# Four reorderings in a fused attention, expert and mixer kernel: GpSimd's splits, the stores of u, one sum of weights, the first means

## The reference, cut to what matters

```python
# 1. attention, 8 heads, 768 tokens, 64 per head: a window of 16 plus 24 block summaries
k_sum = k.reshape(B, H, nb, block, D).max(axis=3)
v_sum = v.reshape(B, H, nb, block, D).mean(axis=3)
a = softmax([masked scale*q@k.T, scale*q@k_sum.T + log(block)])
x = a @ [v, v_sum]
# 2. mixture of 4 experts, each a causal attention of width 64; top 2 by a gate
logits = x @ w_gate;  w = softmax over the two largest
out += w[e] * (softmax(causal(scale * q_e @ k_e.T)) @ v_e @ wo[e])
# 3. mixer
u   = x + (relu(x.T @ w_tok1) @ w_tok2).T
out = u + relu(u @ w_ch1) @ w_ch2
```

## Time and profile before

| what | value |
|---|---|
| median of 3 runs | 450.01 us |
| the profiled execution | 449.9 us, of which the profile spans 448.1 us |
| PE busy | 430.1 us (96%) |
| DVE, ACT, POOL busy | 298.0, 227.8, 134.9 us |
| chain that ended last | PE 85%, DVE 8%, ACT 3%, issue 3% |
| granted clock of PE | 1.00 in every stretch |
| PE idle, 0 to 157 us | 12.75 us |
| PE idle, 157 to 262 us | 1.95 us |

### The profile page before, as it was taken

The page is one execution under the profiler, slowest core; times in us unless marked ns, Lnnn a source line. Parts: engine busy times, 40 slices in busy tenths (PEclk is TensorE's granted clock), DMA queues, the critical chain, the costliest instruction groups (busy, mean ns, idle before and its releaser), DMA issues.

```text
span 448.1 us, 8624 instructions
## 1 busy us (share of the span) xinstructions
PE 430.1 (96%) x3332; PEld 365.2 (81%) x3332; DVE 298.0 (67%) x549; ACT 227.8 (51%) x591; POOL 134.9 (30%) x170
## 2 busy tenths in 40 slices
PE   8889998998997999999999999999999999999997
PEld 3668996787775699968876898988998898989885
DVE  4983489776477834797766977676775775475353
ACT  5884647765247945777783462444442243233120
POOL 3797683000016412000268155632132022200000
PEclk9999999999999999999999999999999999999999
DMA  8964074000582230000033111132123063201103
GB/s 280 345 205 137 3 217 171 1 2 0 187 332 66 50 119 1 0 1 1 1 96 101 41 48 47 48 94 73 41 77 94 1 234 94 78 18 48 47 1 142
DMA packets 14370, 39.69 MB, mean 89 GB/s; under 512 B 1608, under 2 KB 2552, under 8 KB 14328
## 3 DMA queue, kind: packets, MB, share of 16 engines
q1 hardware_dynamic: 13464, 37.55, 25.5%
q10 hardware_dynamic: 864, 1.57, 0.9%
HBM read 33.56 MB, written 4.72 MB: 85 GB/s over the span
## 4 chain that ended last, share of the span: by engine, by line
PE 85%; DVE 8%; ACT 3%; issue 3%; POOL 0%; ACTq 0%; DVEq 0%; POOLq 0%
PE ps_s L690 35%; PE ps_o L690 19%; PE ps_x L690 14%; PE ps_t L690 10%; PE ps_t L862 4%; PE ps_t L757 2%; ACT PA L1101 1%; DVE nmaxM L1451 1%; DVE nmaxA L1359 1%; PE ps_x L876 1%; DVE QS L1399 0%; DVE PTA L1379 0%; DVE PTM L1462 0%; DVE gate_gt L1431 0%; PE ps_s L943 0%
## 5 line engine op out<-in xcount | busy, mean ns | idle before, releaser
L1339 ACT ACTIVATE HID_h<-HID_raw 128x384 fp32r<-128x384 f32 x48 | 25.1, 526 | 72.2 <-DVE HID_raw L1667 32.0
L639 POOL TENSOR_TENSOR W_raw<-W_raw 128x256 f32<-128x256 f32 x11 | 11.7, 1059 | 98.9 <-DMA W_raw<-in_ch 88.2
L1101 ACT ACTIVATE PA<-ps_s,biasA 128x120 f32<-128x120 f32 x96 | 33.6, 377 | 12.7 <-DVE biasA L1363 9.8
L553 POOL TENSOR_TENSOR PA<-PA,denA 128x480 f32<-128x480 f32 x24 | 23.7, 987 | 46.7 <-DVE denA L1372 46.7
L690 PE MATMUL ps_s<-C_h,HID_l 128*128 128x512 f32 x96 | 37.7, 393 | 0.0
L690 PE MATMUL ps_s<-C_l,HID_h 128*128 128x512 f32 x96 | 37.7, 393 | 0.0
L690 PE MATMUL ps_s<-C_h,HID_h 128*128 128x512 f32 x96 | 37.6, 392 | 0.0
L1165 ACT ACTIVATE PM<-ps_s,nmaxM 128x128 f32<-128x128 f32 (+5 forms) x48 | 30.1, 634 | 9.7 <-DVE nmaxM L1451 9.3
L1656 DVE SCALAR_TENSOR_TENSOR HID_l<-HID_raw,HID_h 128x384 fp32r<-128x384 f32 x48 | 28.0, 586 | 10.4 <-ACT HID_h L1339 8.1
L690 PE MATMUL ps_o<-V_h,W_h 128*128 128x384 f32 x96 | 32.8, 342 | 0.1
L690 PE MATMUL ps_o<-V_h,W_l 128*128 128x384 f32 x96 | 32.4, 337 | 0.0
(11 more groups left out here) (255 smaller groups left out, 1265.4 us busy)
## 6 DMA issues: line engine op xcount, KB each, us to landing
VW<-in_vw SPq DMA_DIRECT2D x12, 512.0 KB, 8.3
W_raw<-in_ch SPq DMA_DIRECT2D x12, 512.0 KB, 3.5
C_raw<-in_ch SPq DMA_DIRECT2D x12, 512.0 KB, 3.9
KP<-in_kT SPq DMA_DIRECT2D x8, 384.0 KB, 6.9
VT<-in_vT SPq DMA_DIRECT2D x8, 384.0 KB, 7.3
out_x<-US SPq DMA_DIRECT2D x12, 256.0 KB, 2.1
QT<-in_qT SPq DMA_DIRECT2D x7, 384.0 KB, 6.8
raw<-in_tok SPq DMA_DIRECT2D x4, 384.0 KB, 3.2
```

The lines of the kernel that those rows point to most:

```text
L553: pool.tensor_tensor(PA[:, u % NPA, :, :], PA[:, u % NPA, :, :], denA[:, u % 2, 1, :].unsqueeze(2).broadcast_to([P, 4, KC]), ALU.mult).the ...
L639: pool.tensor_tensor(W[S3], W[A11], W[A21], ALU.subtract).then_inc(w_sum, 1)
L1101: last = act.activation(PA[:, u % NPA, j, :], ps_s[u % 2][:, j % 2, (j // 2) * KC:(j // 2 + 1) * KC], ACT.Exp, bias=biasA[:, u % 4, j:j + ...
L1339: act.activation(*own(s, n, half), ACT.Relu).then_inc(g_hi, 1)
```

## The change

Four edits, none of which adds or removes arithmetic:

1. GpSimd makes splits 3 and 4 (wo, first half of w_tok1) ahead of `no_lows`; splits 5 and 6 stay behind it, and the last split, 7, waits in addition for the whole gate (`m_g` at 12).
2. The six stores of u are issued by SP, among its other DMAs; ACT no longer issues them. Batch 1's `place_means(b, 0, 1)` and `(b, 0, 2)` stand ahead of the fifth store, the three of the second half behind the last.
3. Of the four sums of weights on VectorE the fourth moves behind the low part of the last x.
4. The first means of batch 0 move behind the transposes of unit 0 on PE, and behind the copy of its transposes on ACT.

```diff
+N_EARLY = 5
@@ SP
+            def store_u(b, t):
+                sp.wait_ge(m_u, b * TQ + (t + 1))
+                sp.dma_start(u_d[t * P:(t + 1) * P, :], US1[t][:, :]).then_inc(st_u[t], 16)
...
-                for q in range(2):
-                    for i in range(1 - q, 3):
-                        place_means(b, q, i)
+                for t in range(TQ):
+                    if t == TQ - 2:
+                        for i in (1, 2):
+                            place_means(b, 0, i)
+                    store_u(b - 1, t)
+                for i in range(3):
+                    place_means(b, 1, i)
@@ GpSimd
                 if b == 0:
-                    pool.wait_ge(c_lo, 3)
+                    pool.wait_ge(c_lo, N_EARLY)
...
                 if b == 0:
-                    split(len(PACED))
+                    for n in range(len(PACED), N_EARLY):
+                        split(n)
                 no_lows(b)
                 if b == 0:
-                    for n in range(len(PACED) + 1, N_TOK2):
+                    for n in range(N_EARLY, N_TOK2):
+                        if n == N_TOK2 - 1:
+                            pool.wait_ge(m_g, NGATE)
                         split(n)
@@ PE
+                    if k <= NU + 2:
+                        a_transpose(b, k - 3)
                     if b == 0 and k == 3:
                         a_first_means(b)
-                    if k <= NU + 2:
-                        a_transpose(b, k - 3)
@@ ACT
-            def store_u(b, t):
-                act.wait_ge(m_u, b * TQ + (t + 1))
-                act.dma_start(u_d[t * P:(t + 1) * P, :], US1[t][:, :]).then_inc(st_u[t], 16)
...
+                    if 3 <= k <= NU + 2:
+                        a_to_sbuf(b, k - 3)
                     if b == 0 and k == 3:
                         a_first_means(b)
-                    if 3 <= k <= NU + 2:
-                        a_to_sbuf(b, k - 3)
...
                 for t in range(TQ):
-                    if more:
-                        store_u(b, t)
@@ DVE
                 dve.tensor_tensor(W[S2], W[S1], W[A11], ALU.subtract).then_inc(w_sum1, 1)
+
+            def last_row_sum():
+                W = [W_raw[1][:, a, :, :] for a in range(NB7)]
                 dve.wait_ge(w_sum1, 3)
                 dve.tensor_tensor(W[S4], W[A12], W[S2], ALU.subtract).then_inc(w_sum1, 1)
...
                 if not more:
                     second_row_sums()
                 m_x2_lo(b, TQ - 1)
+                if not more:
+                    last_row_sum()
```

## The result

| what | before | after |
|---|---|---|
| median | 450.01 us | 446.11 us (4 runs, 445.61 to 446.54) |
| ratio, with its 95% interval | | 0.9901 (0.9883 to 0.9919) |
| profiled execution, its span | 449.9, 448.1 us | 445.93, 444.1 us |

By the medians the changed kernel is faster by 3.9 us; the forecast was 3.1. Its median is 0.1 us inside the low end of the range (446.0 to 448.3), while the ratio, applied to 450.01, gives 445.55, a saving of 4.5 us (3.6 to 5.3), just outside that end. The next lines are from the page of the changed kernel: part 1 (busy us, share, count) and, from part 3, the DMA queue of SP. The arithmetic is as before; ACT's queue has no line any more.

A forecast was written before the change was run, and what follows sets the result against it. PE, busy 96% of the span, was taken to bound the kernel. Savings of 1.30 + 1.10 + 0.75 + 0 = 3.15 us off 450.0 gave 446.9 us, with a range of 446.0 to 448.3 us.

The forecast's parts named there:

- Part 1: GpSimd's splits around the gate of batch 0: gate's last instruction 3.90 us earlier, 1.30 us reach PE; bounds 0.6 and 1.7.
- the margin of 1.0 us: Ahead of batch 0's gate: GpSimd's split 6 ends at 57.1 us, the gate starts at 58.08, clear by 1.0.
- The bound of 1.7: Upper bound of the 1.30 us at batch 0's gate, if batch 1's four extra transposes were inside its 14.00 us.
- the four additional transposes of batch 1: Transposes of u on PE, only in batch 1's 14.00 us stretch, compared with batch 0's 15.30 us.
- Part 2: Stores of u off ACT's queue: at the change of batch `normalise` of unit 2 comes 1.10 us earlier; bounds 0.3 and 1.28.
- The rival in which the next wait catches it: Change of batch: full VectorE and GpSimd queues hold unit 3 back, 0.3 of 1.10 arrives, 447.7 us; chance 0.10.
- the stores landing late: Slower rival: u's stores land like SP's loads, `normalise` of unit 2 comes 4.54 us late, 452.5 us; chance 0.02.
- Part 3: VectorE's fourth sum, last x of batch 1: low part starts earlier, PE gains 0.75 us; bounds 0.4 and 0.79.
- Part 4: First means of batch 0: transposes fill PE's 0.67 us gap, VectorE's queue is full; gain 0, bounds -0.3 and 0.3.
- The port lock, a cost of 0: Splits 3 and 4 at 42 to 48.5 us beside VectorE instructions reading PSUM lose nothing to locked ports.
- The stores behind SP's loads, a cost of 0: Stores of u in SP's queue behind batch 1's loads of values: landings as before, 2.0 to 6.1 us after issue.

## Why the prediction was right, and where it was wrong

- **Bound and method.** Right. PE bounds the kernel, each saving was carried to the end once made, and the running difference has no step from 74 to 126 us.
- **Part 1, 1.30 us.** Right in mechanism and size for that execution (1.30, 1.29 and 1.36 in three traces). Two details were off: the margin of 1.0 us was 0.04 where the start came early, and the wait for the gate does nothing. The bound of 1.7 was too low: I took the four additional transposes of batch 1 as the only uncertainty of the 1.30, while the stall itself moves with the phase of two engines, 1.25 to 2.0 us of PE in four traces of the old order.
- **Part 2, 1.10 us.** Right: 1.06. The rival in which the next wait catches it didn't come, nor the stores landing late.
- **Part 3, 0.75 us** measured 0.75 and 0.73. **Part 4, 0** measured 0, for the reason given: VectorE's queue.
- **The port lock, a cost of 0** for the splits moved beside other work of VectorE: right, the running difference doesn't move there. **The stores behind SP's loads, a cost of 0**: right, but from rows read too widely, as said at part 2.
- **The step that failed** is the first one, before any part. PE's gaps were listed "besides the start", which put the start at nothing without a reason, and then came "that is 0.1 us under the median of the runs, so a saving worked out in this trace is taken off 450.0", and with it the range. An execution near the median isn't typical in each of its stretches: this one started late (8.22 us; mean of 14: 7.77), held by fillers that took 6.75 us, and had a cheap stall at the gate (1.30; mean of four: 1.49). The savings themselves were 3.15 us in its own terms and the trace after shows 3.19 for them. What the profiled execution has above that is the start, 0.75 us, for which the sum had no term and the range no room.
- **How far this explains the medians** is argued, not shown, since only a profiled execution shows its start. Three medians of the changed kernel stood 3.9, 3.07 and 3.74 us under those of the kernel before beside them: with the same parts, the size that is measured moves by 0.8 us. The base moved as well: 450.01 came from 3 runs, and later medians of the same kernel were 449.75, 449.65 and 449.91, 0.24 us lower in the mean. An estimate with that base, the counted 3.15 and 0.19 for the dearer stalls gives 446.4, against 446.29 for the mean of the changed kernel's three medians; the 446.11 of the first is luck of its few executions, as far as these runs tell. The likeliest time could not have been known better than by some 0.4 us, and a range whose low end stood 0.9 us under the forecast, all used up by known mechanisms, was too narrow by about that much.

What stays open: what sets the landing of the second load of keys and the moment at which the fillers speed up, and whether the mean saving of the three comparisons, 3.6 us, is above the counted 3.15 by more than chance. Dearer stalls of the old order at the gate would give some 0.2 of it. The first scores start at 7.64 us in the mean of the eight profiles with most of the change and at 7.95 in the other six, a difference that so few profiles with a spread of 1.1 us don't settle.

## What to carry to other kernels

Where two builds run the same matmuls in the same order, subtract the starts of like matmuls: each step of the difference is a place to look for one cause, and what lies in front of the first edited instruction is not the edit's. There, ask what the first useful instruction waits for in each trace: here it was PE's own fillers in one profile and a load in the next. Take the range of a small change from the spread of executions too, at the start and wherever two engines contend by phase, and not from the mechanisms alone. And look behind a gap before closing it: moving GpSimd's maxima gained nothing until VectorE, next in line, had room.

## What the runs showed of the hardware

- The second load of keys lands at 5.36 to 5.61 us in seven profiles and at 5.83 to 6.51 in the other seven, while the first block sums start at 3.93 to 4.34 in all; the same kernel shows both.
- The stall of small VectorE instructions by GpSimd depends on phase: the same twelve instructions took 2.43 us undisturbed, 4.98 us beside the last split alone, and 6.30 to 7.03 us in the old order; the cost to PE ranged from nothing (the 4.98) to 2.0 us (the 7.03).
- PE's 17 fillers of 512 columns, run back to back from 1.54 us, took 5.19 to 6.75 us: they start 0.43 us apart up to a moment between 4.4 and 7.5 us, and 0.22 us apart from then on. The changed kernel alone shows 6.00, 6.44 and 5.29 us.
- The first two stores of u landed in 5.4 to 6.4 us from SP's queue (eight traces) and in 5.3 to 6.2 us from ACT's (six traces), with the loads of values still in flight; the third to sixth landed in 2.0 to 3.8 us from SP's and in 2.0 to 3.5 us from ACT's.
